# Another order of the left-over work beside the first block of a channel MLP

## The chip, the cores and the metric

The kernel runs on one core of a Trainium2 chip. The metric is the device time of one execution in microseconds. Three executions of the kernel before took 1037.57, 1038.95 and 1039.57 us (median 1038.95).

## The reference, cut to what matters

```python
def _moe_ref(x, w_ch1, w_ch2):            # x: (4, 576, 512), the attention's output
    X = np.fft.fft(x, axis=1)
    X = np.fft.fft(X, axis=2)
    mixed = np.real(X).astype(np.float32)
    u = x + mixed
    mu = np.mean(u, axis=-1, keepdims=True)
    var = np.mean((u - mu) ** 2, axis=-1, keepdims=True)
    un = (u - mu) / np.sqrt(var + 1e-06)
    ch = np.maximum(un @ w_ch1, 0.0) @ w_ch2      # w_ch1: (512, 2048), w_ch2: (2048, 512)
    return u + ch

def reference(...):
    attn_out = linear attention with exponential features, batch 4, 8 heads, 576 tokens, 64 per head
    x = attn_out as (4, 576, 512)
    x = _moe_ref(x, ...)
    return _moe2_ref(x, ...)               # a token MLP (576 to 256 to 576), then a channel MLP (512 to 1536 to 512)
```

## The kernel before, in words

All products are made on TensorE from rounded parts: each float32 operand is split into a rounded part (hi) and what is left (lo), and a product takes three passes (hi x hi, hi x lo, lo x hi). The rounding is a copy on ScalarE (ACT); the lo part is a subtraction on VectorE (DVE) or, for the weights, on GpSimd (POOL).

**The front** runs over 16 pairs of heads, four pairs to a batch, and makes attention and then, per batch, the Fourier mixing. The Fourier transform of a real, folded input needs only cosines and sines. A batch has two folds (`fold_s` the sums, `fold_d` the differences, both in the tile `table`). ACT rounds each (`act_fold`, L483), DVE makes its lo part (`dve_low`, L635). Then come eleven pieces of TensorE work (`PIECES`): five over the tokens (three of cosines that read the first fold, two of sines that read the second), then six over the features (cosine and sine in turn, three each). Each piece is written to one of two PSUM banks in turn. A piece over the tokens frees its bank when ACT has rounded it (`act_piece`, L493) and DVE has made its lo part (`dve_piece`, L644); a piece two further on waits for that (`pe_bank_free`). The results of the feature pieces are added to x on POOL: `pool_add` (four instructions, L747 to L751) for each of three parts of a batch, and `pool_row` (two instructions, L757 and L758) for token 288. Before that, ACT copies row 288 of x to a buffer of its own (`act_row`, L473). There is one such buffer, so `act_row` of a batch waits until `pool_row` of the batch before is done. When a batch is whole, SyncE (SP) stores it to DRAM (`store`).

**The first channel MLP** runs over six blocks of 384 tokens, and 16 chunks j of 128 hidden features. For each chunk TensorE does a first product (`pe_first`, 12 matmuls, L983 to L985, into one of two banks) and a second one (`pe_second`, 9 matmuls, L997 to L999). ACT applies the Relu (L1029), DVE makes the lo part (L1097). In a block TensorE's order is first 0, first 1, second 0, first 2, second 1, first 3, second 2, and so on. `pe_first` of chunk j waits for the weights' split j (`w_split`).

**The weights** come one chunk at a time: SP loads 512 KB into one of four raw slots (`load_weights`), ACT rounds them (`act_weights`, L1172), POOL subtracts (`mlp1["gpsimd"]`, L945, 128x1024). A load into a slot waits until POOL has split the chunk that was there.

**Where the two meet.** The first block of the MLP starts before the last batch (LAST, number 3) has been mixed. Its eleven pieces, and the work of the other engines for them, are called from the first block by hand: `tensor_beside`, `scalar_beside`, `vector_beside` say after which step j of the block which piece stands. POOL's order is written out in `gpsimd`: after the last pair's fold it splits the weights 2 and 3, then does the adds that batch 2 has left over (two `pool_add`, one `pool_row`), then the adds of batch 3 with the splits of the further weights between. Every engine works through its own list in order. A wait holds everything behind it on that engine.

Of the kernel before, what the change touches and what calls it, by code (L numbers as in the profile page):

```python
# [64 lines left out]
def wait_if(eng, sem, value):  # L65

    if isinstance(value, int) and value <= 0:
        return
    eng.wait_ge(sem, value)
# [9 lines left out]
def front(nc, ctx, dram, mlp1):  # L79
# [105 lines left out]
    LAST = B - 1  # L185
# [3 lines left out]
    PIECES = [("s", c) for c in range(5)] + [(kind, m) for m in range(FRONT) for kind in ("cos", "sin")]  # L189
# [27 lines left out]
    def load(sp, p):  # L217
        if p.n >= 2:
            sp.wait_ge(qk_split, 2 * p.n - 2)
        sp.dma_start(qk[:, p.parity, KEY], dram["kT"][p.n]).then_inc(k_loaded[p.parity], 16)  # L220
        sp.dma_start(qk[:, p.parity, QUERY], dram["qT"][p.n]).then_inc(q_loaded[p.parity], 16)
        if p.n >= 2:
            sp.wait_ge(kv_done, p.n - 1)
        else:
            sp.wait_ge(ones_set, 4)
        sp.dma_start(v[:, p.parity, :, :, 0:DH], dram["v"][p.n]).then_inc(v_loaded[p.parity], 16)

    def store(sp, b):
        sp.wait_ge(added, FRONT * b + FRONT)
        sp.wait_ge(row_done, b + 1)  # L230
        sp.dma_start(dram["u"][b].rearrange("t p d -> p t d"), x_of(b)).then_inc(u_stored[b], 16)

    def sync(sp):
        sp.dma_start(wphi[:, :], dram["wphi"]).then_inc(consts_loaded, 16)
        sp.dma_start(ident_a[:, :], dram["ident"]).then_inc(consts_loaded, 16)
        load(sp, Pair(0))
        load(sp, Pair(1))
        sp.dma_start(table[:, 0:TCOLS], dram["table"]).then_inc(table_loaded, 16)
        for n in range(2, PAIRS):
            load(sp, Pair(n))  # L240
            if n in (11, 15):
                store(sp, n // 4 - 2)
        sp.wait_ge(qk_split, 2 * PAIRS)
        sp.wait_ge(u_stored[0], 16)
        mlp1["load_block"](sp, 0)
        sp.wait_ge(u_stored[1], 16)
        mlp1["load_early"](sp)
        sp.wait_ge(kv_done, PAIRS)
        sp.wait_ge(qturned, 3 * PAIRS)
        mlp1["load_weights"](sp, 0, [2, 3])  # L250
        sp.wait_ge(x_done, PAIRS)
        mlp1["load_block"](sp, 1)
        mlp1["load_weights"](sp, 4, [0, 1, 2])
        store(sp, 2)
        mlp1["load_weights"](sp, 4, [3])
        mlp1["load_weights"](sp, 8, [0, 1, 2])
        store(sp, 3)
        mlp1["load_weights"](sp, 8, [3])
        mlp1["load_weights"](sp, 12)
        sp.wait_ge(u_stored[2], 16)  # L260
        sp.wait_ge(u_stored[3], 16)
# [116 lines left out]
    def pe_piece(pe, b, i):  # L378

        kind, at_ = PIECES[i]  # L380
        if i >= 2:
            pe_bank_free(pe, b, i - 2)
        elif b > 0:
            pe_bank_free(pe, b - 1, len(PIECES) + i - 2)
        out_bank = four_bank(b, i)
        if kind == "s":
            pe_over_s(pe, b, at_, out_bank)
        elif kind == "cos":
            pe_cosines(pe, b, at_, out_bank)
        else:  # L390
            pe_sines(pe, b, at_, out_bank)
# [33 lines left out]

    def tensor_beside(pe, what, j):

        for i in {("second", 0): (0, 1), ("first", 2): (2, 3), ("second", 1): range(4, len(PIECES))}.get((what, j), ()):
            pe_piece(pe, LAST, i)


# [53 lines left out]
    def act_piece(act, b, i):  # L485

        kind, at_ = PIECES[i]
        if kind == "s":
            rows, n = CHUNKS[at_]
            act.wait_ge(s_done, 5 * b + at_ + 1)  # L490
            if at_ == 0:
                wait_if(act, d_done, 2 * FRONT * b)
            nc.scalar.copy(ab_hi[0:rows, at_, 0:n], four_bank(b, i)[0:rows, 0:n]).then_inc(s_rounded, 1)  # L493
        if kind == "cos":
            q = FRONT * b + at_
            act.wait_ge(d_done, 2 * q + 1)
            wait_if(act, parts_done, q - 1)
            nc.scalar.copy(even[:, q % 2, :], four_bank(b, i)[0:T, 0:FREQ]).then_inc(even_copied, 1)
            if at_ == FRONT - 1:
                wait_if(act, row_done, b)  # L500
                nc.scalar.copy(even288[:, :], four_bank(b, i)[T:T + 1, 0:FREQ]).then_inc(even288_copied, 1)
# [59 lines left out]
    def scalar_beside(act, j):  # L561

        if j == 0:
            mlp1["act_weights"](act, [2])
            act_fold(act, LAST, 0)
            act_fold(act, LAST, 1)
            mlp1["act_weights"](act, [3])
            act_row(act, LAST)
        if j == 1:
            act_piece(act, LAST, 0)  # L570
            act_piece(act, LAST, 1)
            act.wait_ge(fold_split, 2 * B)
            mlp1["act_weights"](act, [4])
        if j == 2:
            for i in range(2, len(PIECES)):
                act_piece(act, LAST, i)
            mlp1["act_weights"](act, [5])
        if j == 3:
            act.wait_ge(d_done, 2 * FRONT * B)
            mlp1["act_weights"](act, [6, 7])  # L580
        if 4 <= j < NF1 - 4:
            mlp1["act_weights"](act, [j + 4])
# [55 lines left out]
    def dve_piece(dve, b, i):  # L638

        kind, at_ = PIECES[i]  # L640
        if kind == "s":
            rows, n = CHUNKS[at_]
            dve.wait_ge(s_rounded, 5 * b + at_ + 1)
            nc.vector.tensor_tensor(ab_lo[0:rows, at_, 0:n], four_bank(b, i)[0:rows, 0:n], ab_hi[0:rows, at_, 0:n],  # L644
                                    ALU.subtract).then_inc(s_split, 1)
        if kind == "sin":
            q = FRONT * b + at_
            src = four_bank(b, i)[0:T, 0:FREQ]
            dve.wait_ge(even_copied, q + 1)
            dve.wait_ge(d_done, 2 * q + 2)  # L650
            wait_if(dve, added, q - 2)
            nc.vector.tensor_tensor(less[:, q % 3, :], even[:, q % 2, :], src, ALU.subtract)
            nc.vector.tensor_tensor(more[:, q % 3, :], even[:, q % 2, :], src, ALU.add).then_inc(parts_done, 1)
# [43 lines left out]
    def vector_beside(dve, j):  # L697

        if j == 0:
            dve_low(dve, LAST, 0)  # L700
            dve_low(dve, LAST, 1)
        if j == 1:
            dve_piece(dve, LAST, 0)
            dve_piece(dve, LAST, 1)
        if j == 2:
            for i in range(2, len(PIECES)):
                dve_piece(dve, LAST, i)
        if j == 9:
            dve.wait_ge(row_done, B)
# [31 lines left out]
    def pool_add(pool, b, m):  # L741
        q = FRONT * b + m
        if m == 0:
            pool.wait_ge(rows_kept, b + 1)
        pool.wait_ge(parts_done, q + 1)
        out = x_of(b)[:, m, :]
        nc.gpsimd.tensor_tensor(out[:, 0:257], out[:, 0:257], less[:, q % 3, 0:257], ALU.add)  # L747
        nc.gpsimd.tensor_tensor(out[:, 257:D], out[:, 257:D], more[:, q % 3, 255:0:-1], ALU.add)
        out = x_of(b)[:, FRONT + m, :]
        nc.gpsimd.tensor_tensor(out[:, 0:257], out[:, 0:257], more[:, q % 3, 0:257], ALU.add)  # L750
        nc.gpsimd.tensor_tensor(out[:, 257:D], out[:, 257:D], less[:, q % 3, 255:0:-1], ALU.add).then_inc(added, 1)  # L751

    def pool_row(pool, b):
        pool.wait_ge(even288_copied, b + 1)
        pool.wait_ge(added, FRONT * b + FRONT)
        out = x_of(b)[0:1, FRONT, :]
        nc.gpsimd.tensor_tensor(out[:, 0:257], row288[:, 0:257], even288[:, 0:257], ALU.add)  # L757
        nc.gpsimd.tensor_tensor(out[:, 257:D], row288[:, 257:D], even288[:, 255:0:-1], ALU.add).then_inc(row_done, 1)  # L758
# [21 lines left out]
    def gpsimd(pool):  # L780
        pool_split(pool, Pair(0))
        for k in range(-1, PAIRS):
            pool_step(pool, k)
        pool_fold(pool, Pair(PAIRS - 1))
        mlp1["gpsimd"](pool, (), 2, 4)
        pool_add(pool, LAST - 1, 1)
        pool_add(pool, LAST - 1, 2)
        pool_row(pool, LAST - 1)
        pool_add(pool, LAST, 0)
        pool.wait_ge(d_done, 2 * FRONT * B)  # L790
        mlp1["gpsimd"](pool, (), 4, 6)
        pool_add(pool, LAST, 1)
        mlp1["gpsimd"](pool, (), 6, 7)
        pool_add(pool, LAST, 2)
        pool_row(pool, LAST)
        mlp1["gpsimd"](pool, ((7, u_stored[2], 16), (13, u_stored[3], 16)), 7)
# [735 lines left out]
```

## Time and profile before

| | |
|---|---|
| profiled execution, its own time | 1037.23 us |
| its span, first to last instruction | 1035.4 us |
| runs, median (lowest, highest) | 1038.95 us (1037.57, 1039.57) |
| PE busy | 1011.9 us, 98% of the span |
| DVE, ACT, POOL busy | 391.8, 290.4, 188.1 us |
| mean granted TensorE clock | 0.992 |

PE is TensorE's matmuls, PEld its weight loads. Times of rows are microseconds from the start of the span. A granted clock of 1.00 is 2.4 GHz, 0.50 is 1.2 GHz. The first block of the first channel MLP runs from about 222 to 315 us; the place of the change lies between 226 and 257 us.

### The profile page before, as it was taken

What the parts mean: (1) busy time and instruction counts of PE and PEld (TensorE: products, weight loads), DVE (VectorE), ACT (ScalarE), POOL (GpSimd) and SP (SyncE); (2) the same over time, 40 slices, a digit from 0 to 9 for tenths busy, and PEclk for the clock granted to TensorE, in tenths of its full rate; (3) what the DMA queues carried; (4) which work ended last, traced back from release to release, by engine and by line L of the source; (5) the groups of instructions that cost most, each with busy time, mean ns of one, the idle gap of its engine ahead of it and who ended that gap; (6) DMA issues with size and microseconds to landing.
All of it is one profiled execution on the core that took longest, in us unless ns stands there. A gap on an engine that the chain in (4) does not pass through costs nothing.

```text
span 1035.4 us, 18136 instructions
## 1 busy us (share of the span) xinstructions
PE 1011.9 (98%) x7731; PEld 905.3 (87%) x7731; DVE 391.8 (38%) x690; ACT 290.4 (28%) x580; POOL 188.1 (18%) x159
## 2 busy tenths in 40 slices
PE   7999999997999999999999999999999999999998
PEld 5999898986999999999999999777889899999997
DVE  5697878882142231222222213545121212121211
ACT  5765555652331111111111113243111111111110
POOL 2552735474930000000000000053100000000000
PEclk9999999998999999999999999999999999999999
DMA  5322232332601001010010120576101010101000
GB/s 174 97 81 66 73 119 73 132 134 66 191 18 62 1 31 31 1 61 0 0 61 0 48 52 1 168 242 225 46 1 61 1 62 1 61 0 61 0 32 30
DMA packets 47649, 66.34 MB, mean 64 GB/s; under 512 B 22432, under 2 KB 23392, under 8 KB 47456
## 3 DMA queue, kind: packets, MB, share of 16 engines
q1 hardware_dynamic: 45856, 59.10, 18.2%
q10 hardware_dynamic: 1728, 6.29, 1.7%
q8 instruction: 51, 0.84, 0.3%
q14 instruction: 14, 0.11, 0.0%
HBM read 46.51 MB, written 18.87 MB: 63 GB/s over the span
## 4 chain that ended last, share of the span: by engine, by line
PE 91%; DVE 4%; POOL 3%; ACT 1%; issue 1%; DMA 0%; SPq 0%; DVEq 0%; ACTq 0%; POOLq 0%
PE mlp_y L998 11%; PE mlp_y L999 11%; PE mlp_hid L985 11%; PE mlp_hid L983 11%; PE mlp_hid L984 11%; PE mlp_y L997 11%; PE num L316 3%; PE kv L302 3%; PE proj L273 2%; PE four L322 1%; PE proj L274 1%; PE proj L275 1%; PE mlp_turn_in L968 1%; PE four L325 1%; PE tok_y L1262 1%; PE four L324 1%
## 5 line engine op out<-in xcount | busy, mean ns | idle before, releaser
L1097 DVE SCALAR_TENSOR_TENSOR mlp_h_lo<-mlp_hid,mlp_h_hi 128x384 fp32r<-128x384 f32 x168 | 93.7, 558 | 468.6 <-ACT mlp_h_hi L1029 468.6
L983 PE MATMUL mlp_hid<-mlp_ut_hi,mlp_w_hi 128*128 128x384 f32 x672 | 229.2, 341 | 0.0
L985 PE MATMUL mlp_hid<-mlp_ut_hi,mlp_w_lo 128*128 128x384 f32 x672 | 226.5, 337 | 0.0
L984 PE MATMUL mlp_hid<-mlp_ut_lo,mlp_w_hi 128*128 128x384 f32 x672 | 225.5, 336 | 0.0
L1029 ACT ACTIVATE mlp_h_hi<-mlp_hid 128x384 fp32r<-128x384 f32 x168 | 82.6, 492 | 501.1 <-PE mlp_hid L985 501.1
L999 PE MATMUL mlp_y<-mlp_w_hi,mlp_h_lo 128*128 128x512 f32 x504 | 199.6, 396 | 0.0
L998 PE MATMUL mlp_y<-mlp_w_lo,mlp_h_hi 128*128 128x512 f32 x504 | 199.1, 395 | 0.0
L997 PE MATMUL mlp_y<-mlp_w_hi,mlp_h_hi 128*128 128x512 f32 x504 | 197.6, 392 | 0.4 <-DVE mlp_h_lo L1097 0.2
L945 POOL TENSOR_TENSOR mlp_w_lo<-mlp_w_raw,mlp_w_hi 128x1024 fp32r<-128x1024 f32 x26 | 62.5, 2421 | 409.8 <-DVE tok_x_lo L1317 396.5
L983 PEld LDWEIGHTS mlp_hid<-mlp_ut_hi,mlp_w_hi 128*128 128x128 f32 x672 | 126.3, 188 | 5.7 <-DVE mlp_ut_lo L1083 0.2
L984 PEld LDWEIGHTS mlp_hid<-mlp_ut_lo,mlp_w_hi 128*128 128x128 f32 x672 | 126.3, 188 | 5.3
L985 PEld LDWEIGHTS mlp_hid<-mlp_ut_hi,mlp_w_lo 128*128 128x128 f32 x672 | 126.0, 188 | 0.0
L999 PEld LDWEIGHTS mlp_y<-mlp_w_hi,mlp_h_lo 128*128 128x128 f32 x504 | 94.6, 188 | 20.4
L997 PEld LDWEIGHTS mlp_y<-mlp_w_hi,mlp_h_hi 128*128 128x128 f32 x504 | 95.0, 188 | 16.0 <-issue 0.5
L998 PEld LDWEIGHTS mlp_y<-mlp_w_lo,mlp_h_hi 128*128 128x128 f32 x504 | 94.8, 188 | 16.0
L589 DVE TENSOR_REDUCE absmax<-proj 128x4 f32<-128x512 f32 (+1 forms) x80 | 50.5, 632 | 35.3 <-PE proj L275 35.1
L716 POOL TENSOR_TENSOR qk_lo<-qk,qk_hi 128x576 fp32r<-128x576 f32 x32 | 46.1, 1444 | 96.6 <-ACT qk_hi L436 96.6
L273 PE MATMUL proj<-wphi_hi,qk_hi 128*128 128x256 f32 x144 | 48.7, 338 | 10.1 <-DVE pm L597 6.2
L463 ACT ACTIVATE eq<-pt 128x512 f32<-128x512 f32 (+1 forms) x96 | 42.0, 490 | 50.1 <-PE pt L288 43.6
L597 DVE TENSOR_TENSOR pm<-proj,absmax 128x512 f32<-128x512 f32 (+1 forms) x80 | 51.1, 638 | 5.1 <-ACT ek L449 0.5
L1083 DVE TENSOR_TENSOR mlp_ut_lo<-mlp_turn_in,mlp_ut_hi 128x384 fp32r<-128x384 f32 x44 | 24.5, 558 | 73.6 <-ACT mlp_ut_hi L1022 73.4
L449 ACT ACTIVATE ek<-pm 128x512 f32<-128x512 f32 (+1 forms) x96 | 48.4, 558 | 4.4 <-DVE pm L597 4.4
(123 smaller groups left out, 1166.4 us busy)
## 6 DMA issues: line engine op xcount, KB each, us to landing
mlp_u<-u_scratch SPq DMA_DIRECT2D x12, 768.0 KB, 4.6
mlp_w_raw<-in_w_mlp SPq DMA_DIRECT2D x14, 512.0 KB, 4.4
mlp_w_raw<-in_w_mlp ACTq DMA_DIRECT2D x12, 512.0 KB, 7.1
v<-in_v SPq DMA_DIRECT2D x16, 320.0 KB, 3.7
qk<-in_kT SPq DMA_DIRECT2D x16, 288.0 KB, 4.0
qk<-in_qT SPq DMA_DIRECT2D x16, 288.0 KB, 4.0
u_scratch<-x_all SPq DMA_DIRECT2D x4, 1152.0 KB, 6.6
x_scratch<-mlp_u SPq DMA_DIRECT2D x5, 768.0 KB, 3.6
```

The lines of the kernel that those rows point to most:

```text
L273: nc.tensor.matmul(out, hi, wphi_hi[:, :], start=True, stop=False)
L589: nc.vector.tensor_reduce(absmax[:, unit, 0:cols], src, AX.X, ALU.max, apply_absolute_value=True).then_inc(absmax_done, 1)
L597: nc.vector.tensor_tensor(pm[p.parity][:, unit, 0:cols, :], src, top, ALU.subtract).then_inc(shifted, 1)
L945: nc.gpsimd.tensor_tensor(w_lo[:, nf - 1 - j, :], raw(j), w_hi[:, j, :], ALU.subtract).then_inc(w_split, 1)
L983: nc.tensor.matmul(out, w_hi[:, j, col], hi, start=(c == 0), stop=False)
L984: nc.tensor.matmul(out, w_hi[:, j, col], lo, start=False, stop=False)
L985: last = nc.tensor.matmul(out, w_lo[:, nf - 1 - j, col], hi, start=False, stop=(c == DC - 1))
L997: nc.tensor.matmul(y[t][:, :], hi, w_hi[:, j, D:2 * D], start=(j == 0), stop=False)
L998: nc.tensor.matmul(y[t][:, :], hi, w_lo[:, nf - 1 - j, D:2 * D], start=False, stop=False)
L999: last = nc.tensor.matmul(y[t][:, :], lo, w_hi[:, j, D:2 * D], start=False, stop=(j == nf - 1))
L1029: nc.scalar.activation(h_hi[:, j % 2, :], hid[j % 2][:, 0:BT], ACT.Relu).then_inc(h_rounded, 1)
L1097: nc.vector.scalar_tensor_tensor(out=h_lo[:, j % 2, :], in0=hid[j % 2][:, 0:BT], scalar=0.0, in1=h_hi[:, j % 2, :], op0=ALU.max, op1=ALU.s ...
```

## The change

All of it lies in the front's lists for the last batch:

- TensorE does the five token pieces in one go after `second 0`, and the six feature pieces after `second 1`. Before, two stood after `second 0`, two after `first 2` and seven after `second 1`.
- ACT rounds both folds first and then the weights 2 and 3; before, weights 2 stood ahead of the folds and weights 3 behind. The copy of row 288 moves from the end of step 0 to step 1, behind the rounding of the five token pieces.
- DVE follows with the pieces: five in step 1, six in step 2.
- POOL does the left-over adds of batch 2 ahead of the splits of weights 2 and 3.
- SP stores batch 2 ahead of the load of weights 6 (slot 2), no longer behind it.

```diff
@@ sync
-        mlp1["load_weights"](sp, 4, [0, 1, 2])
+        mlp1["load_weights"](sp, 4, [0, 1])
         store(sp, 2)
-        mlp1["load_weights"](sp, 4, [3])
+        mlp1["load_weights"](sp, 4, [2, 3])
@@ tensor_beside
-        for i in {("second", 0): (0, 1), ("first", 2): (2, 3), ("second", 1): range(4, len(PIECES))}.get((what, j), ()):
+        for i in {("second", 0): range(5), ("second", 1): range(5, len(PIECES))}.get((what, j), ()):
             pe_piece(pe, LAST, i)
@@ scalar_beside
         if j == 0:
-            mlp1["act_weights"](act, [2])
             act_fold(act, LAST, 0)
             act_fold(act, LAST, 1)
-            mlp1["act_weights"](act, [3])
+            mlp1["act_weights"](act, [2, 3])
+        if j == 1:
+            for i in range(5):
+                act_piece(act, LAST, i)
             act_row(act, LAST)
-        if j == 1:
-            act_piece(act, LAST, 0)
-            act_piece(act, LAST, 1)
             act.wait_ge(fold_split, 2 * B)
             mlp1["act_weights"](act, [4])
         if j == 2:
-            for i in range(2, len(PIECES)):
+            for i in range(5, len(PIECES)):
                 act_piece(act, LAST, i)
             mlp1["act_weights"](act, [5])
@@ vector_beside
         if j == 1:
-            dve_piece(dve, LAST, 0)
-            dve_piece(dve, LAST, 1)
+            for i in range(5):
+                dve_piece(dve, LAST, i)
         if j == 2:
-            for i in range(2, len(PIECES)):
+            for i in range(5, len(PIECES)):
                 dve_piece(dve, LAST, i)
@@ gpsimd
         pool_fold(pool, Pair(PAIRS - 1))
-        mlp1["gpsimd"](pool, (), 2, 4)
         pool_add(pool, LAST - 1, 1)
         pool_add(pool, LAST - 1, 2)
         pool_row(pool, LAST - 1)
+        mlp1["gpsimd"](pool, (), 2, 4)
         pool_add(pool, LAST, 0)
         pool.wait_ge(d_done, 2 * FRONT * B)
         mlp1["gpsimd"](pool, (), 4, 6)
```

## Rows read from the trace of the kernel before

**Rows 1.** Page, busy time of each engine, share of the span, instructions

```profile
PE 1011.9 (98%) x7731; PEld 905.3 (87%) x7731; DVE 391.8 (38%) x690; ACT 290.4 (28%) x580; POOL 188.1 (18%) x159
```

**Rows 2.** Waits of PE, 200 to 420 us: total, times, longest

```profile
PE four L322 <- DVE ab_lo L644: 6.8, 1, 6.8
PE four L322 <- DVE fold_lo L635: 1.3, 1, 1.3
```

**Rows 3.** Windows: length; busy PE, PEld, DVE, ACT, POOL; clock; DMA share; GB/s

```profile
235.75:242.50 6.75, 0.00 (x0) 0.00 (x0) 0.95 (x3) 1.98 (x5) 4.54 (x7) 0.68 0.17 51
242.50:248.30 5.80, 5.77 (x22) 4.55 (x23) 1.80 (x4) 1.71 (x4) 0.00 (x0) 0.50 0.82 234
```

**Rows 4.** Timeline, ACT: start, duration, line, operation, tiles, [idle before, releaser]

```profile
226.47 1.04 ACT L1172 CAST mlp_w_hi<-mlp_w_raw 128x1024 fp32r<-128x1024 f32 x1
227.41 1.58 ACT L483 CAST fold_hi<-table 97x774 fp32r<-97x774 f32 x2
...
240.52 0.62 ACT L473 COPY row<-x_all 1x512 f32<-1x512 f32 x1 [10.59 <-POOL x_all L758]
...
247.06 0.40 ACT L493 CAST ab_hi<-four 128x288 fp32r<-128x288 f32 x1 [1.77 <-PE four L325]
```

**Rows 5.** Timeline, POOL

```profile
226.54 1.01 POOL L738 TENSOR_TENSOR table<-table 96x384 f32<-96x384 f32 x1
227.59 5.48 POOL L945 TENSOR_TENSOR mlp_w_lo<-mlp_w_raw,mlp_w_hi 128x1024 fp32r<-128x1024 f32 x2
233.03 1.36 POOL L747 TENSOR_TENSOR x_all<-x_all,less 96x257 f32<-96x257 f32 x1
...
236.11 0.74 POOL L747 TENSOR_TENSOR x_all<-x_all,less 96x257 f32<-96x257 f32 x1
...
270.95 9.48 POOL L945 TENSOR_TENSOR mlp_w_lo<-mlp_w_raw,mlp_w_hi 128x1024 fp32r<-128x1024 f32 x4
```

**Rows 6.** Timeline, DVE

```profile
228.35 5.54 DVE L635 TENSOR_TENSOR fold_lo<-table,fold_hi 97x774 fp32r<-97x774 f32 x2 [1.19 <-ACT fold_hi L483]
...
247.49 0.46 DVE L644 TENSOR_TENSOR ab_lo<-four,ab_hi 128x288 fp32r<-128x288 f32 x1 [1.72 <-ACT ab_hi L493]
```

**Rows 7.** Line 635: duration in ns (min/median/max), first and last start

```profile
L635 DVE TENSOR_TENSOR fold_lo<-table,fold_hi x8: 950/1221/3149, 74.5 to 230.7; 97x774 fp32r<-97x774 f32 x4, 96x774 fp32r<-96x774 f32 x4
```

**Rows 8.** Timeline, PE: second 0's last matmul; starts of groups of matmuls

```profile
229.23 0.39 PE L999 MATMUL mlp_y<-mlp_w_hi,mlp_h_lo 128*128 128x512 f32 x1
...
249.66 0.30 PE L322 MATMUL four<-table_hi,fold_hi 96*128 96x288 f32 x1
...
250.88 0.28 PE L322 MATMUL four<-table_hi,ab_hi 128*96 128x258 f32 x1
...
256.88 0.34 PE L983 MATMUL mlp_hid<-mlp_ut_hi,mlp_w_hi 128*128 128x384 f32 x1
...
261.05 0.33 PE L983 MATMUL mlp_hid<-mlp_ut_hi,mlp_w_hi 128*128 128x384 f32 x1
...
273.61 0.34 PE L983 MATMUL mlp_hid<-mlp_ut_hi,mlp_w_hi 128*128 128x384 f32 x1
```

**Rows 9.** Timeline, PE: two earlier waits, in the front

```profile
125.06 0.36 PE L273 MATMUL proj<-wphi_hi,qk_hi 128*128 128x256 f32 x1 [2.23 <-DVE pm L597]
...
181.58 0.35 PE L273 MATMUL proj<-wphi_hi,qk_hi 128*128 128x256 f32 x1 [2.23 <-DVE pm L597]
```

**Rows 10.** Windows around these two, PE alone: length, busy, clock, DMA share, GB/s

```profile
125.00:130.00 5.00, 4.95 (x37) 0.66 0.00 2
...
180.00:185.00 5.00, 3.22 (x23) 1.00 0.01 3
```

**Rows 11.** Page, DMA issues: tiles, queue, count, KB each, us to landing

```profile
mlp_w_raw<-in_w_mlp SPq DMA_DIRECT2D x14, 512.0 KB, 4.4
...
u_scratch<-x_all SPq DMA_DIRECT2D x4, 1152.0 KB, 6.6
```

## The prediction, made before the changed kernel ran

> **What bounds the kernel now.** I read the page's busy times first: PE is busy for 98% of the span [rows 1]. Shares of other engines therefore matter only where PE waits. The list of PE's waits shows where that is beside this change: two waits only, 6.8 us for DVE's `ab_lo` and 1.3 us for DVE's `fold_lo` [rows 2]. The windows show that the long one costs more than itself. Within its 6.75 us PE did nothing and the granted clock averaged 0.68, so it fell on the way; for the next 5.80 us, with PE busy, it stayed at 0.50, the lower level of 1.2 GHz [rows 3]. That stretch lost half of 5.80, or 2.9 us.
>
> The timelines say why. ACT's queue stood still for 10.59 us in front of the copy of row 288, which waits for POOL's last `x_all` add of batch 2 [rows 4]. Everything behind it stood too: the Relu of chunk 1 and the rounding of Fourier pieces 0 and 1. DVE could not make `ab_lo`, so no bank came free for piece 2, and PE stopped. POOL was late because it did two weight splits (227.59, 5.48 us) ahead of the adds, which began at 233.03 and let ACT go at 240.52 [rows 4, 5]. The 1.3 us wait comes from DVE: two `fold_lo` took 5.54 us beside the weight splits [rows 6], against 0.95 us at the best [rows 7].
>
> **The change part by part.** I follow it up to the first matmul of `first 3`, at 256.88 now [rows 8]. From there the lists of both kernels are the same, so what PE gains by then it should keep.
>
> *ACT's folds first.* The rounding of fold 0 takes the place of a weight copy at 226.47 and is done at about 227.3 (half of 1.58); fold 1 waits for POOL's difference, done at 226.54 + 1.01 = 227.55, and ends near 228.4 [rows 4, 5]. This is 1 us earlier than now. The two weight copies come behind it, 1.04 us each, to 230.5. They hold up only the Relu of chunk 1 and piece 0, whose matmuls take until then anyway.
>
> *POOL: adds first.* They begin at 227.59. From the first add's start to ACT's release they took 240.52 − 233.03 = 7.49 us, in which one add was lengthened by a collision with the second `fold_lo` (1.36 against 0.74 us, so 0.62) [rows 4, 5]. Without any collision this is 6.9 us; with both `fold_lo` in it 8.1 us. DVE's two roundings now fall right into the adds, so I take 8.1: POOL has finished batch 2 at 235.7. Then the split of weights 2: 9.48 / 4 = 2.37 us undisturbed, 2.74 beside `fold_lo` [rows 5]. DVE has nothing like it left by then, so 2.37: done at 238.1, with 0.1 for the signal 238.2. Weights 3 follow at 240.5.
>
> The collision itself shows in the rows: `fold_lo` takes 2.8 us on average beside splits of 2.74 us, and the add beside it gets longer by 0.62 [rows 5, 6]. The Trainium skill ("SBUF — State Buffer", section "Who interferes with whom") speaks against putting the adds beside the folds: a VectorE instruction with two inputs in SBUF contends with a GpSimd instruction that reads SBUF, and the later of the two is blocked for a whole instruction. By that rule each `fold_lo` waits for at most one add and each holds up one add, which gives the 8.1 us; without it the sum would go by 6.9. The trace agrees, with the 0.62 us of one add.
>
> *DVE.* `fold_lo` 0 starts at 227.4 (now 228.35 [rows 6]), waits for POOL's current instruction and ends near 228.4; `fold_lo` 1 near 229.8. Both come before PE needs them.
>
> *PE.* `second 0` ends at 229.23 + 0.23 = 229.46 and piece 0 follows at once: the 1.3 us wait is gone. A token piece takes 250.88 − 249.66 = 1.22 us [rows 8]. A bank comes free by a rounding on ACT and a subtraction on DVE, from 247.06 to 247.95, 0.9 us with PE's last matmul just before [rows 4, 6]; the other bank's piece covers 1.22 us of that. So five pieces end at 229.46 + 6.1 = 235.6, perhaps half a microsecond later through ACT's weight copies. This costs nothing, because of what is late next: `first 2` needs the split of weights 2, at 238.2. PE waits 2.6 us there, a wait that the kernel before doesn't have. Up to 2.6 us of slowness of the pieces hides in it.
>
> *After that.* `first 2` and `second 1` take 261.05 − 256.88 = 4.17 us, the six feature pieces 256.88 − 250.88 = 6.00 [rows 8]. `first 3` starts at 238.2 + 10.2 = 248.4 with the clock at 2.4 GHz throughout. Its weights 3 are ready since 240.5. The gain is 256.88 − 248.4 = 8.5 us.
>
> *The clock.* PE's waits of 2.23 us at 125 and at 181 us went either way: after the first the clock averaged 0.66 over 5 us, after the second it stayed at 1.00 [rows 9, 10]; the long one brought it down [rows 3]. A wait of 2.6 us lies between, nearer to those that sometimes fall. If it falls, I price it by the first: (1 − 0.66) x 5 = 1.7 us; 2.9 us is the dear end [rows 3]. I hold a fall for likelier than none: gain 8.5 − 1.7 = 6.8 us.
>
> *SP.* The store of batch 2 goes out at 235.8 instead of 240.5, and the load of weights 6, which it now precedes, waits for the split of weights 2. The load could start at 238.2 and, even with the whole of a store ahead, land at 238.2 + 6.6 + 4.4 = 249.2 [rows 11]. ACT rounds weights 6 after `first 3` and the Relu of chunk 3, past 250.5. So no cost. *The copy of row 288* stands behind the pieces and finds POOL done (235.7) when ACT gets to it near 236. Moves of DVE's pieces cost nothing beyond what is counted.
>
> *The weights behind.* POOL starts weights 4 when the last feature piece is done, as before. The tightest place is weights 7: the first of the four splits at 270.95 ends at 273.32, and `first 7` starts at 273.61 [rows 5, 8]. Both move along with the pieces' end, so the 0.3 us stays; I allow 0.3 us of loss and take none.
>
> **The sum.** The profiled execution took 1037.23 us, its span is 1035.4, and 1.8 us lie around it. 1037.23 − 6.8 = 1030.4. The three runs' median is 1.7 above this execution and would give 1032.2. I take 1031.2, between the two.
>
> Ends: with no collision POOL is done at 234.5 and weights 2 at 236.9, PE waits 1.3 us, the gain is 9.8 us: 1027.4. At the other end each `fold_lo` costs POOL its whole 0.95 us and the split takes 2.74: 227.59 + 6.9 + 1.9 + 2.74 + 0.1 = 239.2, a gain of 7.5, less 2.9 for the clock: 4.6, or 1034.3 from the runs' median.
>
> **The rivals.**
>
> *The clock holds.* The same wait of 2.6 us, but as at 181 us no fall: gain 8.5, 1028.7 from the profiled execution, 1030.5 from the median. For it: one of two waits of 2.23 us; against it: this one is longer.
>
> *POOL is quick.* `fold_lo` slips between instructions at no cost to the adds, the 1.3 us wait at `first 2` is too short for a fall: gain 9.8, 1027.4 to 1029.2. Against it: the lengthened add in the rows.
>
> *Slower: DVE doesn't get past POOL's adds.* The place is `fold_lo` 0 at 227.4. If POOL's waiting instructions always went first, DVE would start only when POOL runs dry: 227.59 + 6.9 + 2 x 2.37 = 239.2. PE would then stand from 229.46 to 240.2, start with a low clock (2.9 us lost), need 6.1 + 10.2 us, and be at `first 3` at 259.4, against 256.88 now: 2.5 us slower, 1039.7 to 1041.5. It decides from a `fold_lo` that ends past about 237.6. Against it: the second `fold_lo` of now ended at 228.35 + 5.54 = 233.9, with POOL's adds still queued and running until 240.5.
>
> *No change: the wait only moves.* If ACT's two weight copies, now ahead of the Relu of chunk 1 and all pieces, had to wait for their load, the pieces would be held as now. It takes some 10 us of delay to get back to 256.88, and both copies ran without a wait at 226.47 and after the folds [rows 4].
>
> **How the numbers follow.** Forecast (wait at `first 2`, with a fall) 0.50; the clock holds 0.27; POOL is quick 0.15; no change 0.04; slower 0.04. 0.2%, or 2.1 us, is about what a measurement of this kernel can tell from no change. The first three are all faster by more: 0.92 faster, 0.04 same, 0.04 slower. Range 1028.0 to 1033.6: it holds the forecast and the held clock from either base and most of the quick case, and leaves the dear end and the last two out.
>
> **What would show it.** In the changed profile: no wait of PE for `fold_lo` before piece 0, or one far below 1.3 us; five token pieces in a row from 229.5; ACT's copy of row 288 with under 1 us of idle ahead; POOL's batch 2 done near 235.7; PE's one wait, 2.6 us, at L983 for POOL's `mlp_w_lo`; `first 3` near 248.4, or 250.1 with a stretch at 0.50. The prediction is wrong if PE's wait is for `ab_lo` or `fold_lo` again, if new waits on `mlp_w_lo` come after `first 3`, or if the second half of the kernel gives the gain back.

## The result, and the profile after

The changed kernel took 1031.01 us (median of 4 runs, 1030.49 to 1031.78), the kernel before on the same chip 1038.4. The ratio is 0.9932, 95% interval 0.992 to 0.9944: 7.4 us less. The forecast was 1031.2, the range 1028.0 to 1033.6.

The profiled execution took 1031.78 us, its span is 1029.9. That is 5.5 us less than the span before and not 7.4, and the cause lies ahead of the change. At the start of the kernel, where both programs are the same, the clock was low for longer in this execution. PE's first matmul after 16 us starts at 16.08 us before and at 16.04 after; a later one of the same lists starts at 30.83 and at 31.87. The windows of PE alone (length, busy, clock, DMA share, GB/s), before and then after:

```profile
15.00:20.00 5.00, 3.92 (x20) 0.66 0.03 12
20.00:25.00 5.00, 5.00 (x105) 1.00 0.09 20
```

```profile
15.00:20.00 5.00, 3.96 (x18) 0.51 0.04 15
20.00:25.00 5.00, 5.00 (x96) 0.81 0.01 3
```

Lost by the clock, that is (0.66 − 0.51 + 1.00 − 0.81) x 5 = 1.7 us more. By `second 0` the changed kernel's times are 1.40 us later than the other's (its last matmul starts at 230.63, against 229.23 [rows 8]). I therefore measure the change from that matmul to the first of `first 3`.

PE's waits between 200 and 420 us, after (total, times, longest):

```profile
PE mlp_hid L982 <- POOL mlp_w_lo L944: 2.4, 1, 2.4
PE mlp_y L996 <- DVE mlp_h_lo L1096: 0.2, 1, 0.2
```

Both waits of [rows 2] are gone; a new one stands at `first 2`, for POOL's split of weights 2. PE's timeline shows piece 0, the last matmul of piece 4, and then the starts of `first 2`, of the feature pieces and of `first 3`:

```profile
230.87 0.30 PE L322 MATMUL four<-table_hi,fold_hi 97*128 97x290 f32 x1
...
236.84 0.29 PE L325 MATMUL four<-table_hi,fold_lo 96*128 96x288 f32 x1
239.56 0.41 PE L982 MATMUL mlp_hid<-mlp_ut_hi,mlp_w_hi 128*128 128x384 f32 x1 [2.43 <-POOL mlp_w_lo L944]
...
245.34 0.28 PE L322 MATMUL four<-table_hi,ab_hi 128*96 128x258 f32 x1
...
251.36 0.34 PE L982 MATMUL mlp_hid<-mlp_ut_hi,mlp_w_hi 128*128 128x384 f32 x1
```

From `second 0`'s last matmul to `first 3` it is 251.36 − 230.63 = 20.73 us, against 256.88 − 229.23 = 27.65 [rows 8]: 6.92 us less. Nothing is given back behind it: `first 3` starts 5.52 us earlier than before, and the span is 5.5 us shorter.

The timelines of POOL, ACT and DVE after, in this order, answer to [rows 4 to 6]:

```profile
228.91 0.64 POOL L746 TENSOR_TENSOR x_all<-x_all,less 96x257 f32<-96x257 f32 x1
229.50 1.35 POOL L747 TENSOR_TENSOR x_all<-x_all,more 96x255 f32<-96x255 f32 x1
230.82 1.36 POOL L749 TENSOR_TENSOR x_all<-x_all,more 96x257 f32<-96x257 f32 x1
...
237.07 4.68 POOL L944 TENSOR_TENSOR mlp_w_lo<-mlp_w_raw,mlp_w_hi 128x1024 fp32r<-128x1024 f32 x2
...
265.39 9.45 POOL L944 TENSOR_TENSOR mlp_w_lo<-mlp_w_raw,mlp_w_hi 128x1024 fp32r<-128x1024 f32 x4
```

```profile
227.98 0.84 ACT L483 CAST fold_hi<-table 97x774 fp32r<-97x774 f32 x1
229.04 0.84 ACT L483 CAST fold_hi<-table 96x774 fp32r<-96x774 f32 x1 [0.22 <-POOL table L737]
...
237.46 0.61 ACT L473 COPY row<-x_all 1x512 f32<-1x512 f32 x1
```

```profile
228.93 2.75 DVE L634 TENSOR_TENSOR fold_lo<-table,fold_hi 97x774 fp32r<-97x774 f32 x2 [0.36 <-ACT fold_hi L483]
```

The two `fold_lo` take 2.75 us instead of 5.54. Two of POOL's adds were lengthened, one for each. ACT comes to the row copy with POOL already done and doesn't wait. The weights' split starts at 237.07; taken back by the 1.40 us that is 235.67 in the times of the kernel before. The windows of PE alone show the clock after the new wait:

```profile
235.00:240.00 5.00, 2.57 (x19) 1.00 0.39 110
240.00:245.00 5.00, 5.00 (x19) 0.66 0.97 306
245.00:250.00 5.00, 5.00 (x37) 1.00 0.07 30
```

### The profile page after: what moved, and what is told of

It is laid out like the page before. It is cut to its first block, busy times and chain, and to the rows that moved or that the text cites. A ratio compares the mean times of both kernels' runs of the same rounds, so it can differ in the third digit from the quotient of the medians.

```text
span 1029.9 us, 18136 instructions
## 1 busy us (share of the span) xinstructions
PE 1011.4 (98%) x7731; PEld 905.8 (88%) x7731; DVE 389.6 (38%) x690; ACT 290.9 (28%) x580; POOL 188.0 (18%) x159
## 4 chain that ended last, share of the span: by engine, by line
PE 91%; DVE 4%; POOL 3%; ACT 1%; issue 1%; DMA 0%; SPq 0%; DVEq 0%; ACTq 0%; POOLq 0%
PE mlp_hid L984 11%; PE mlp_hid L982 11%; PE mlp_y L997 11%; PE mlp_y L998 11%; PE mlp_hid L983 11%; PE mlp_y L996 11%; PE num L316 3%; PE kv L302 3%; PE proj L273 2%; PE proj L275 1%; PE proj L274 1%; PE mlp_turn_in L967 1%; PE four L322 1%; PE tok_y L1261 1%; PE pt L288 1%; PE four L325 1%
```

## The experiments

The theory: PE had stood because ACT's queue stood in front of the row copy; the change takes that wait away and leaves one of 2.4 us for weights 2, plus a fall of the clock. The rival: POOL's earlier adds alone make the gain. "Stretch" is the time from `second 0`'s last matmul to `first 3` in the profile of a kernel (before 27.65, after 20.73 us). Times are medians; the kernel before had 1037.8, 1038.03, 1037.86 and 1037.67 us beside the four groups of runs. Each group had a chip of its own, so medians of different groups compare to about half a microsecond.

**The row copy back ahead of the pieces** (from the changed kernel):

```diff
             mlp1["act_weights"](act, [2, 3])
+            act_row(act, LAST)
         if j == 1:
             for i in range(5):
                 act_piece(act, LAST, i)
-            act_row(act, LAST)
```

> The changed kernel with one part undone: ACT copies row 288 at the end of step 0 again, ahead of the Relu of chunk 1 and of the roundings of the five token pieces. Theory (ACT's queue): the gain comes from ACT no longer standing in front of the row copy with the pieces behind it. POOL lets the copy go at about 237.1 in the changed kernel's times, so piece 0 is rounded near 238.2, piece 2 starts near 239.0 instead of 233.3, and PE waits 5.7 us for DVE's ab_lo instead of 2.4 us for POOL's weights 2. With 3.7 us of pieces, 4.2 us of MLP and 6.0 us of pieces behind it, and 1.7 to 2.9 us for the clock, first 3 starts at 254.6 to 255.8 instead of 251.4: 1034.2 to 1035.4 us. Rival (POOL's order): the gain comes from the earlier adds alone, the copy's place matters little: 1031 to 1032 us.

Measured 1035.57 us, stretch 24.84. Its list of PE's waits has the one for `ab_lo` again:

```profile
PE four L322 <- DVE ab_lo L643: 5.7, 1, 5.7
```

Its timeline of ACT shows the queue standing in front of the copy:

```profile
236.98 0.62 ACT L473 COPY row<-x_all 1x512 f32<-1x512 f32 x1 [5.36 <-POOL x_all L757]
```

This is the theory's wait, to the tenth; the time is 0.2 us above its range. The copy's place is needed even with POOL's early adds.

**POOL's order back** (weights 2 and 3 ahead of the adds, SP's store behind the load of weights 6; from the changed kernel):

```diff
+        mlp1["gpsimd"](pool, (), 2, 4)
         pool_add(pool, LAST - 1, 1)
         pool_add(pool, LAST - 1, 2)
         pool_row(pool, LAST - 1)
-        mlp1["gpsimd"](pool, (), 2, 4)
```

> The changed kernel with POOL's order undone (splits of weights 2 and 3 ahead of the left-over adds again, and SP's store behind the load of weights 6). Theory (ACT's queue): no loss. Weights 2 are split before PE comes to first 2, so the wait of 2.4 us there goes; ACT's row copy now waits for the adds until some 5 us after piece 4 is rounded, and holds the Relu of chunk 2 and the copy of the first cosine piece, so PE waits about 2 us in the feature pieces, on ab_lo's banks' other users (ACT's even or DVE's parts). Time 1029.0 to 1030.7 us by whether the clock falls. Rival (POOL's order): the adds are as late as in the kernel before, most of the gain goes: 1036 us or more.

Measured 1029.7 us (1028.21 to 1033.16), stretch 18.19. The runs spread with the mean clock: 0.997 in the fastest, 0.990 in the slowest. The rival falls: without POOL's new order the kernel is no slower. In its timeline ACT waits 4.93 us at the copy, but has rounded the token pieces by then:

```profile
243.62 0.62 ACT L473 COPY row<-x_all 1x512 f32<-1x512 f32 x1 [4.93 <-POOL x_all L757]
```

In its list of waits PE loses 1.4 us to that, where 2 were expected:

```profile
PE four L322 <- ACT even L498: 1.4, 1, 1.4
```

**POOL's order alone** (from the kernel before, the same lines the other way, and SP's):

> The kernel before with POOL's order (and SP's) of the change alone. Theory (ACT's queue): the row copy still stands ahead of pieces 0 and 1 but goes about 4.8 us earlier; in exchange first 2 waits for weights 2 until about 238.2 in the times of the kernel before, PE's waits are about 5.9 us in one instead of 1.3 and 6.8, the clock falls all the same. Gain 2 to 3 us: 1035.2 to 1036.4 us. Rival (POOL's order): nearly the whole gain, 1031 to 1032 us.

Measured 1035.7 us, stretch 25.03, as the theory had it: 2.1 us of gain. In its list of PE's waits, those of 1.3 and 6.8 us became one of 5.7:

```profile
PE mlp_hid L983 <- POOL mlp_w_lo L945: 5.7, 1, 5.7
```

**POOL's work interleaved** (from the changed kernel; SP's order as before the change):

```diff
         pool_add(pool, LAST - 1, 1)
+        mlp1["gpsimd"](pool, (), 2, 3)
         pool_add(pool, LAST - 1, 2)
         pool_row(pool, LAST - 1)
-        mlp1["gpsimd"](pool, (), 2, 4)
+        mlp1["gpsimd"](pool, (), 3, 4)
```

> The changed kernel with POOL's left-over work in another order: first add, split of weights 2, second add and row, split of weights 3 (and SP's loads of weights 4 to 6 ahead of the store, as in the kernel before). Theory (the new wait at first 2 is all that is left): weights 2 are ready at about 234.8 in the changed kernel's times, before PE comes to them at 237; the row is free near 238.7 and weights 3 near 241.1, both before PE needs what hangs on them. PE has no wait between the folds and first 3, the clock does not fall: 2.4 + 1.7 us less, 1026.9 us. Rival (POOL's amount of work sets the time): the wait only moves to the row copy or to weights 3, 1030 to 1031 us.

Measured 1026.57 us (1026.2 to 1027.3), ratio to the kernel before 0.9888 (0.9874 to 0.9902), stretch 16.52: 4.4 us faster than the changed kernel and the best of all. The list of PE's waits from 190 to 420 us has only the old one of 0.2 us:

```profile
PE mlp_y L997 <- DVE mlp_h_lo L1097: 0.2, 1, 0.2
```

Its timelines of POOL (split of weights 2) and ACT (row copy):

```profile
232.49 2.39 POOL L945 TENSOR_TENSOR mlp_w_lo<-mlp_w_raw,mlp_w_hi 128x1024 fp32r<-128x1024 f32 x1
```

```profile
239.30 0.62 ACT L473 COPY row<-x_all 1x512 f32<-1x512 f32 x1 [1.96 <-POOL x_all L757]
```

Weights 2 are ready at 234.9, and PE comes to `first 2` at 236.7, so the wait of 2.4 us and the low clock behind it are gone. SP's order went back in the same run and was not undone alone; PE has no wait that hangs on it. ACT's 1.96 us at the copy cost nothing: nothing that PE needs soon stands behind it.

**TensorE's order back** (from the changed kernel):

```diff
-        for i in {("second", 0): range(5), ("second", 1): range(5, len(PIECES))}.get((what, j), ()):
+        for i in {("second", 0): (0, 1), ("first", 2): (2, 3), ("second", 1): range(4, len(PIECES))}.get((what, j), ()):
```

> The changed kernel with TensorE's order undone: two token pieces after second 0, two after first 2, the rest after second 1. Theory (PE's list): first 2 waits for the split of weights 2, and three pieces no longer stand ahead of it to use that time: PE waits about 6.1 us there instead of 2.4 us, and the 3.7 us of pieces come behind. With the clock at its low level for 1.7 us more or less, 3.7 to 4.9 us slower than the changed kernel: 1034.7 to 1035.9 us. Rival (only ACT's list counts, PE's order is free): 1031 us.

Measured 1035.89 us, stretch 25.21. Five pieces in one go are worth 4.9 us here. Three of them fill the time that PE waits for weights 2: without them the wait is 6.0 us and not 2.4. This holds beside POOL's new order, which makes weights 2 late; with POOL's old order the part was not undone alone. So the 4.6 us of the row copy's place and these 4.9 us don't add up: each is worth that much only beside the rest. Its list of PE's waits:

```profile
PE mlp_hid L982 <- POOL mlp_w_lo L944: 6.0, 1, 6.0
PE four L322 <- ACT even L498: 0.6, 1, 0.6
```

**The folds' order back** (weights 2 ahead of the folds again; from the changed kernel):

> The changed kernel with ACT's fold order undone: weights 2 ahead of the folds, weights 3 behind. Theory (covered): fold 0 is rounded 1 us later, DVE's first fold_lo ends about when PE comes to piece 0, which may wait up to 0.5 us; the wait of 2.4 us for weights 2 shortens by the same. Time 1031 us, within 0.5. Rival (folds first is part of the gain): the 1.3 us wait of the kernel before comes back on top: 1032.3 us.

Measured 1030.92 us, stretch 20.73, the same as with the folds first. No wait for `fold_lo` came back; its list of PE's waits has the one for weights 2:

```profile
PE mlp_hid L983 <- POOL mlp_w_lo L945: 2.1, 1, 2.1
```

Beside the rest of the change this part is worth nothing.

**The new wait filled** (from the changed kernel; the products are not read):

```diff
             pe_piece(pe, LAST, i)
+        if (what, j) == ("second", 0):
+            for _ in range(15):
+                nc.tensor.matmul(proj[1][:, 0:HALF], fold_hi[0:T, 1, 0, 0:128], table_hi[0:T, TS:TS + HALF],
+                                 start=True, stop=True)
```

> The changed kernel with 15 more matmuls of 96x288 after the five token pieces, whose result nothing reads: about 2.0 us of TensorE work put into the wait of 2.4 us before first 2. They add work and take no wait away. Theory (the clock's price): PE's wait shrinks to 0.4 us, first 2 starts at the same time, the clock stays at 2.4 GHz, and the 1.7 us that it cost afterwards come back: 1029.3 us. Rival (the low clock costs nothing, the stretch behind is bounded by POOL): 1031.0 us, or more for the added work.

Measured 1029.4 us (1029.01 to 1030.01, all below the changed kernel's 1030.49 to 1031.78), stretch 19.24. The wait shrank to 0.5 us and the clock didn't fall. In the medians 1.6 us came back, in the stretch 1.5. The window of PE after the wait:

```profile
240.00:245.00 5.00, 5.00 (x29) 1.00 0.93 311
```

More work, and faster: this is the price of the fall. (The 95% intervals of the two ratios to the kernel before, 0.9901 to 0.9926 and 0.992 to 0.9944, overlap at their ends.)

**The row copy alone** (from the kernel before):

```diff
             mlp1["act_weights"](act, [3])
-            act_row(act, LAST)
         if j == 1:
             act_piece(act, LAST, 0)
             act_piece(act, LAST, 1)
+            act_row(act, LAST)
```

> The kernel before with one line moved: ACT's copy of row 288 stands behind the roundings of pieces 0 and 1 and no longer ahead of the Relu of chunk 1. POOL's, PE's and SP's order as before. Theory (ACT's queue): this alone gives over half of the gain. ACT still waits for POOL's adds until 240.5, but pieces 0 and 1 are rounded by then, so PE goes on through first 2, pieces 2 and 3 and second 1 to about 240.0 and waits there for piece 2's rounding, until about 243.5: one wait of 3.5 us instead of 6.8. first 3 at 250.8, or 252.5 with a fall of the clock, instead of 256.9: 1031.7 to 1033.5 us. Rival (POOL's order): the adds end when they did, so the time stays at 1037 to 1038 us.

Measured 1038.89 us (1033.8 to 1040.46), ratio 1.0003 (0.999 to 1.0015): no gain, a miss for the theory as I had put it. In its list of waits PE's are as expected, the long one with its end at 243.69:

```profile
PE four L322 <- DVE ab_lo L644: 3.3, 1, 3.3
PE four L322 <- DVE fold_lo L635: 1.3, 1, 1.3
```

But the clock behind it was not, by the windows of PE alone:

```profile
245.00:250.00 5.00, 5.00 (x24) 0.53 0.50 161
250.00:255.00 5.00, 5.00 (x22) 0.50 0.00 0
255.00:260.00 5.00, 5.00 (x19) 0.60 0.20 41
```

From 245.3 to 259.0 PE was busy without a gap, and the clock stayed at 0.50 through the six feature pieces and `first 3`. That is 13.7 us at 1.2 GHz, 6.8 us lost, against 2.9 behind the longer wait of the kernel before; `second 2` starts at 259.04 against 258.96 before. The twelve runs go with the clock: the two fastest (1033.8 and 1034.44 us) have a mean clock of 0.993, the other ten, from 1037.31 us on, 0.985 to 0.990. The next three kernels test this.

**Its wait filled** (24 matmuls as above, ahead of piece 4):

> The kernel before with the row copy alone moved (row_alone), and 24 more matmuls of 96x288, whose result nothing reads, ahead of piece 4: 3.2 us of TensorE work in its wait of 3.3 us. In row_alone the wait was where theory put it, first piece 4 at 243.7, but the clock fell at 245.3 and stayed at 0.50 to 259.0, through all six feature pieces: 13.6 us at half the clock, 6.8 us lost, which is the whole of the gain that failed. Theory (clock): with the wait filled the clock does not fall, first 3 starts near 250.9 instead of 255.2 and the 6.8 us come back: 1032 us. Rival (the row copy's place is worth nothing, something else gives the time back): 1038 to 1039 us.

Measured 1032.76 us, stretch 21.61: 6.1 us faster than `row_alone`, with 24 matmuls more. The window behind the filled wait, where `row_alone` had 0.53:

```profile
245.00:250.00 5.00, 5.00 (x38) 1.00 0.56 176
```

The clock costs the missing gain: without its fall the time lies in the range that the theory gave for `row_alone`.

**Dense products behind the wait** (10 matmuls of 128x512, not read, between piece 4 and the feature pieces):

> row_alone with 10 more matmuls of 128x512, whose result nothing reads, between piece 4 and the six feature pieces, behind the wait, not in it: work added, 2.2 us at 2.4 GHz, 4.3 us at 1.2 GHz. Theory (after a fall, PE's clock comes back in dense products and not in the feature pieces): the clock falls at the same place, rises again during or just after the added matmuls, and the feature pieces and first 3 run at 2.4 GHz: 4.3 us more work, 10.2 - 6.0 = 4.2 us of feature pieces and 1.7 us of first 3 less, 1037 us, 1 to 2 us faster than row_alone in spite of the added work, and a low stretch of 3 to 5 us instead of 13.6. Rival (the low stretch has its length whatever PE does, or the feature pieces bring the clock down again): 1041 to 1043 us, the low stretch as long as before.

Measured 1036.71 us (1034.07 to 1038.54): its median is 2.2 us below that of `row_alone` in spite of the added work, which is the theory's direction, but the intervals of the two ratios overlap (0.9979 to 0.9997, and 0.999 to 1.0015). In the profiled execution (1034.07 us) the clock didn't fall at all after the same wait of 3.3 us, so the trace doesn't show what the dense products did after a fall. A fall that comes in fewer of the runs would give the time as well. The theory is not tested by this kernel.

**Second 1 behind the wait** (from `row_alone`):

```diff
-        for i in {("second", 0): (0, 1), ("first", 2): (2, 3), ("second", 1): range(4, len(PIECES))}.get((what, j), ()):
+        for i in {("second", 0): (0, 1), ("first", 2): (2, 3, 4), ("second", 1): range(5, len(PIECES))}.get((what, j), ()):
```

> row_alone with one piece moved in TensorE's list: piece 4, which waits, stands ahead of second 1 and no longer behind it. No work is added. The waiting gets longer by second 1's 2.1 us, to 5.4 us, with the same end at 243.5; behind it come piece 4, second 1 and then the six feature pieces. Theory (a low clock is cheap where MLP products follow the wait and dear where the feature pieces follow it): the clock falls, is back before or soon after the end of second 1, a low stretch of 4 to 6 us instead of 13.6; first 3 near 255: 1035 to 1036.5 us, faster than row_alone in spite of 2.1 us more of waiting. Rival (the low stretch is as long as it was, or the feature pieces themselves bring the clock down): first 3 near 258 to 260: 1039.5 to 1041 us.

Measured 1037.16 us (1034.58 to 1037.59), 0.7 us above the theory's range and 2.3 below the rival's. The median is 1.7 us below that of `row_alone`, with a wait 2.1 us longer; again the intervals overlap (0.9979 to 0.9996, and 0.999 to 1.0015). The wait was 5.36 us, and the clock fell inside it, at 243.7, not behind it as in `row_alone`. The windows of PE show its return near 250.6, at the end of `second 1`, and the feature pieces (from 250.82) at 2.4 GHz:

```profile
245.00:250.00 5.00, 5.00 (x16) 0.50 0.73 218
250.00:255.00 5.00, 5.00 (x33) 0.94 0.00 0
```

**The old wait filled** (from the kernel before, 48 matmuls ahead of piece 2, not read):

> The kernel before with 48 more matmuls of 96x288, whose result nothing reads, ahead of piece 2: 6.4 us of TensorE work in its wait of 6.8 us. Theory (clock's price): the clock does not fall, the 5.8 us at 0.50 behind the wait cost 2.9 us less: 1035.1 us. Rival (that stretch was bounded by ACT and DVE, not by PE's clock): 1038 us.

Measured 1036.14 us (1034.65 to 1042.1), between the two. In the profile the stretch was 25.02, 2.6 us shorter, with a wait of 0.4 us left and no low clock behind it. That is the price of the old fall in this one execution. Over the runs the median is 1.7 us lower, not clear of noise: the ratio is 0.9987 (0.9974 to 1.0). The one run of 1042.1 us had a mean clock of 0.990 where the other ten had 0.995 to 0.997; it has no trace that would say where.

This kernel and `row_alone_filled` give the row copy's place without the clock: in both the long wait is filled and the clock stays at 1.00 behind it. They differ by 3.4 us in the medians (1036.14 and 1032.76) and by 3.4 in the stretch (25.02 and 21.61). The two waits, 6.8 and 3.3 us, differ by 3.5.

## Why the prediction was right, point by point

- *What bounds the kernel*: confirmed. ACT's queue in front of the row copy held PE; `row_back` brings the wait back. POOL's new order without the rest isn't enough: in `pool_alone` the two old waits give way to one of 5.7 us at `first 2`, and the gain is 2.1 us.
- *POOL done with batch 2 at 235.7, with both `fold_lo` in the adds*: 237.07 − 1.40 = 235.67. The choice of the dear end (8.1 us of adds) was right: from 228.91 to 237.07 it is 8.16 us, with the adds of 1.35 and 1.36 us in it. Here the rule of the Trainium skill ("SBUF — State Buffer", section "Who interferes with whom") agrees with the trace: one add for each `fold_lo`.
- *PE's wait at `first 2` of 2.6 us*: 2.43. The last matmul of the five pieces starts at 236.84 − 1.40 = 235.44 and ends at 235.73, where 235.6 was said; the split of weights 2 took 2.34 us, half of 4.68.
- *The clock falls and costs 1.7 us*: it fell once PE was busy again, and averaged 0.66 over 5 us, 1.7 us. `wait_filled` gives 1.6 us for the whole fall. That the clock would fall was a choice between two waits that went either way, and nothing here settles it better: waits of 3.3 us brought the clock down in the profile of `row_alone` and not in that of `row_alone_dense`. This half of the hit is luck.
- *`first 3` at 250.1 with a fall*: 251.36 − 1.40 = 249.96. *Gain 6.8 us*: 6.92 in the stretch, 7.4 between the medians.
- *The sum between two bases (1030.4 and 1032.2)*: the profiled execution before (1037.23) lay 0.4 to 0.8 us under the medians of the later groups of runs, and the first median (1038.95) above them, so the middle, 1038.0, was a fair base. Beside the changed kernel the one before took 1038.4. The base was 0.4 us too low and the gain, 6.8 against 7.4, 0.6 too small; the two misses nearly cancel, so that the forecast came within 0.2 us of the time is partly luck.
- *Weights 7 keep their 0.3 us*: the split ends at 265.39 + 9.45 / 4 = 267.75, and `first 7` starts at 268.09. No wait.
- *Folds first, 1 us earlier, hidden*: right that it hides. `folds_back` shows that the 1.3 us wait stays away without it, by POOL's new order, and `pool_alone`, with the folds in the old order, has none either; `pool_back` has no such wait either, because behind the folds the rounding of weights 2 and 3 comes late and POOL's splits begin only at 232.06. Either edit is enough.
- *POOL's order*: I counted it as what the change needs. `pool_back` shows that it isn't: 1029.7 us against 1031.0 (the intervals of the two ratios overlap), with a stretch 2.5 us shorter in the profile, of which 1.7 us is the clock, which did not fall there. Once the copy stands behind the pieces, late adds cost PE 1.4 us, and weights 2 are what PE needs first. I had worked out where the new wait would be and didn't ask whether the old order would have had it.
- *The rivals*: the slower one fell at its own mark: both `fold_lo` had ended at 231.68 − 1.40 = 230.3, far from 237.6, between POOL's adds. POOL was not quick: its adds took 8.16 us and not 6.9. The clock did not hold in the profile. No part moved the wait back.

The clock's price was right for this place, but the prediction gave it as the price of a wait of this length. `row_alone` shows a wait of 3.3 us with a price of 6.8 us. Here MLP products follow the wait, there the feature pieces do; that this makes the difference is argued and not shown. Had I priced that move alone, I would have been wrong by the whole gain.

## What to carry to other kernels

When one queue stands in front of a wait, first move what others need from behind it; then ask which of the waits left ends last, and give that work its place by deadline (weights 2 between the adds, 4.4 us), not all of one kind ahead of the other. A wait of TensorE can cost more than its length: in these traces a wait of a few microseconds was followed by no low clock, or by one that cost 1.7, 2.9 or 6.8 us, so give its price as a range. A part of a change that looks like its core can be worth nothing: undo each alone.

## What the runs showed of the hardware that I had not expected

After a wait the clock's low stretch was not of one length. PE worked at 1.2 GHz for 3.4 us in the changed kernel (240.4 to 243.8, in `first 2` and `second 1`), for 5.7 us in `row_alone_second` (244.9 to 250.6, piece 4 and `second 1`), for 5.7 us in `row_back` (239.0 to 244.7, token pieces) and for 5.9 us in the kernel before (242.5 to 248.5; [rows 3] shows the first 5.8 of them). In `row_alone` it was 13.7 us, from 245.3 to 259.0, without an idle gap: the six feature pieces, among them products with a single row of weights, and `first 3`. In three of these kernels the clock had fallen within the wait already; counted from there the low stretch was 6.8 us in `row_alone_second` (from 243.7) and in `row_back` (from 237.8) and 10.2 us in the kernel before (from 238.2). So the feature pieces stood behind the longest one, but it is a single trace, and nothing here shows that they are the reason; why is open.

The clock also fell when PE was busy again: in `row_alone` at 245.3, 1.6 us after the wait's end, and in the changed kernel at 240.4, 0.8 us after it. And added work that filled a wait lowered the median in three of three cases, by 1.6, 6.1 and 1.7 us; of these the 6.1 us are clear of noise by the intervals, the 1.6 by runs that don't overlap, the 1.7 not.
